# Three 128x9 and 128x4 products move from VectorE to GpSimd, and the splitting of weight parts moves to the end of GpSimd's round

## Chip, core and metric

One core of a Trainium2 chip runs the whole program in one launch. The metric is the device time of that launch in microseconds (us), the median of several runs. The engines are called as in the profile: PE (TensorE; PEld is its weight load), DVE (VectorE), ACT (ScalarE), POOL (GpSimd) and SP (SyncE, which issues the DMAs).

## What is computed

```python
# attention with a memory, B, H, S, D = 4, 8, 576, 64
scores = q @ k^T / sqrt(D), causal
a = exp(scores - max);  a /= a.sum(-1) + 1e-9
local = a @ v
q_p = phi(q)                        # phi(x) = (x if x > 0 else exp(x) - 1) + 1
mem_out = (q_p @ M_prev) / (q_p . z_prev + 1e-6)
g = 1 / (1 + exp(-beta))
x = g * mem_out + (1 - g) * local   # laid out as 2304 tokens x 512
# two dense blocks, d_model 512, d_ff 2048
x = act1(x @ w_in1) @ w_out1        # act1: 0 below -1, h above 1, (h + 1)^2 / 4 between
x = act2(x @ w_in2) @ w_out2        # act2(h) = h * sigmoid(h)
```

## The kernel before

The program has two stages. The first is the attention: 16 rounds, one for each pair of heads p (two heads side by side on the 128 partitions). The second is the two dense blocks, in which PE multiplies in three passes (high and low parts of the operands). No scheduler is at work: each engine's program is written out by hand, and semaphores join them.

**A round of attention.** In round p PE first turns (transposes) the probabilities of pair p: `turn_both` twice and `turn_corner`, nine products at L899 that open the round. Then it forms the scores of pair p+1 (L862), turns more blocks (eleven products at L899, which reuse the PSUM banks of scores), turns phi and the row weights (`turn_rest` with L933 and L934, then `turn_phi` and `turn_row`), and ends with the values and the memory product. The eleven products may start once DVE has taken the maximum of the first scores of pair p+1 out of PSUM (`s_read`).

**DVE's part of iteration p**: the row weights of pair p (`rows`, L674 to L687), `to_x(p-1)` (L711: finished sums times row weight, from PSUM into X), a copy (L704), the masked maxima of pair p+1 (L653), the low parts `klo` (L627) and `qlo` (L635) of pair p+2, and the norms of phi of pair p+1 (`norms`, L659 to L668). All are in that order, so what is late in `rows` delays `to_x` and the maxima behind it.

**The two weights.** With den the row sum of the exponentials (L674), the kernel scales by 1/den only at the end, so phi's weight is den * g / norm. `norms` makes norm (L659), its reciprocal (L664) and times g (L668). `rows` makes den, its reciprocal (L680), den times that share (L685, `rw[:, 1]`), and for the last 64 rows of both heads the small table `rwt` (L687).

**POOL's round p**: `phi_sum_1(p+1)` (L353), `weigh(p)` (L386 and L389: phi times its weight into `phs`), `widen(p)` (L377, L379), in some rounds `split_part` of a weight matrix part (L335, L337), `phi_sum_2` (L358), the high parts `khi` (L344) and `qhi` (L348) of pair p+2, phi times z (L363), and the values times 1 - g (L371). `parts_beside` places one part in each of the rounds 5, 7, 9, 11, 13 and 14 and two in round 15; the other 56 parts are split in the dense stage. A part lands from SP's queue (`fetch`) in one of three slots of `stage`.

Of the kernel before, what the change touches and what calls it, by code (L numbers as in the profile page):

```python
# [7 lines left out]
ALU = mybir.AluOpType  # L8
# [3 lines left out]
P = 128  # L12
# [5 lines left out]
def build(nc, qT, kT, qN, vN, mN, zN, bN, w_in1, w_out1, w_in2, w_out2, out):  # L18
# [6 lines left out]
    PAIRS = NPAIR // B  # L25
    FULL = S // P
# [16 lines left out]
    NB = 2 * FULL + 1  # L43
# [9 lines left out]
    with ExitStack() as ctx:  # L53
        def sem(name):
            return ctx.enter_context(nc.semaphore(name))

        def sb(name, shape, dt=F32, where=ctx):
            return where.enter_context(nc.sbuf_tensor(name, shape, dt))
# [14 lines left out]
        att = ExitStack()  # L73
# [27 lines left out]
        rwide = sb("rwide", [P, 2 * FULL + 2, D], where=att)  # L101
        rwt = sb("rwt", [P, 2, 2], where=att)
        mden = sb("mden", [P, 2, NB], where=att)
        qn = [sb(f"qn{i}", [P, NB, D], where=att) for i in range(2)]
        phie = [sb(f"phie{i}", [P, NB, D + 1], where=att) for i in range(2)]
        phir = [sb(f"phir{i}", [P, NB, D], where=att) for i in range(3)]
# [80 lines left out]
        hi_done, lo_done = sem("hi_done"), sem("lo_done")  # L187
        phi_part, phi_sum, phi_norm = sem("phi_part"), sem("phi_sum"), sem("phi_norm")
        norm_step, row_step, row_wide = sem("norm_step"), sem("row_step"), sem("row_wide")
        weighed, v_done = sem("weighed"), sem("v_done")  # L190
        s_full, s_read, exp_done = sem("s_full"), sem("s_read"), sem("exp_done")
        t_full, ev_act, ev_dve = sem("t_full"), sem("ev_act"), sem("ev_dve")
# [40 lines left out]
        def parts_beside(p):  # L233
            return [u for u, at in enumerate(PARTS_AT) if at == p]
# [92 lines left out]
        def _(pool):  # L327
            def split_part(u):
                layer, f, half = parts[u]
                if layer == 0 and f == EARLY and half == 0:  # L330
                    pool.wait_ge(x_free, NPAIR + 1)
                if layer == 1 and half == 0:
                    pool.wait_ge(g_free, (TILES - 1) * FC + f + 1)
                landed(pool, u)
                nc.gpsimd.tensor_copy(W[f][:, 2 * half, :], stage[:, u % 3, :]).then_inc(w_hi, 1)  # L335
                pool.wait_ge(w_hi, u + 1)
                nc.gpsimd.tensor_tensor(W[f][:, 2 * half + 1, :], stage[:, u % 3, :],  # L337
                                        W[f][:, 2 * half, :].bitcast(F32), ALU.subtract).then_inc(w_split, 1)
# [11 lines left out]
            def phi_sum_1(p):  # L350
                pool.wait_ge(phi_part, 2 * p + 2)
                both = phir[p % 3]
                nc.gpsimd.tensor_tensor(both[:], qn[p % 2][:], both[:], ALU.add).then_inc(phi_sum, 1)  # L353
# [20 lines left out]
            def widen(p):  # L374
                if p:
# [3 lines left out]
                nc.gpsimd.tensor_copy(rwide[:, 0:2 * FULL, :], rw[:, 0, 0:2 * FULL].unsqueeze(2)  # L379
                                      .broadcast_to([P, 2 * FULL, D])).then_inc(row_wide, 1)  # L380

            def weigh(p):
                pool.wait_ge(row_step, 4 * p + 4)
                if p:
                    pool.wait_ge(t_full, TURNS * (p - 1) + T_PHI + 1)
                nc.gpsimd.tensor_tensor(phs[:, 0:2 * FULL, :], phir[p % 3][:, 0:2 * FULL, :],  # L386
                                        rw[:, 1, 0:2 * FULL].unsqueeze(2).broadcast_to([P, 2 * FULL, D]),
                                        ALU.mult).then_inc(weighed, 1)
                nc.gpsimd.tensor_tensor(phs[:, 2 * FULL:, :], phir[p % 3][:, 2 * FULL:, :].broadcast_to([P, 2, D]),  # L389
                                        rwt[:, 1, :].unsqueeze(2).broadcast_to([P, 2, D]),  # L390
                                        ALU.mult).then_inc(weighed, 1)
# [35 lines left out]
            for p in range(NPAIR):  # L427
                if 0 < p < NPAIR - 1:
                    phi_sum_1(p + 1)
                weigh(p)  # L430
                widen(p)

                for u in parts_beside(p):
                    split_part(u)

                if 0 < p < NPAIR - 1:
                    phi_sum_2(p + 1)
                if p + 2 < NPAIR:
                    high_k(p + 2)
                    high_q(p + 2)  # L440
                if p + 1 < NPAIR:
                    phi_times_z(p + 1)
                    weigh_v(p + 1)
            for u in range(2 * EARLY, 4 * FC):
                split_part(u)

# [2 lines left out]
        def _(act):  # L449
# [12 lines left out]
            def phi_part_2(p):  # L462
                act.wait_ge(phi_part, 2 * p + 1)
                if p >= 2:
                    act.wait_ge(norm_step, 3 * p - 5)
                nc.scalar.activation(phie[p % 2][:, :, 0:D], phir[p % 3][:], ACT.Exp, scale=-1.0).then_inc(phi_part, 1)

            def split_x(layer, tile, k_):
# [152 lines left out]
        def _(dve):  # L621
# [34 lines left out]
            def norms(p, step):  # L656
                if step == 0:
                    dve.wait_ge(phi_norm, p + 1)
                    nc.vector.tensor_reduce(mden[:, 0], phie[p % 2][:], AX.X, ALU.add).then_inc(norm_step, 1)  # L659
                elif step == 1:  # L660
                    dve.wait_ge(norm_step, 3 * p + 1)
                    if p:
                        dve.wait_ge(row_step, 4 * p - 1)
                    nc.vector.reciprocal(mden[:, 1], mden[:, 0]).then_inc(norm_step, 1)  # L664
                else:
                    dve.wait_ge(norm_step, 3 * p + 2)
                    dve.wait_ge(gate_step, 5)
                    nc.vector.tensor_tensor(mden[:, 1], mden[:, 1], gcols[:, p % PAIRS, :],  # L668
                                            ALU.mult).then_inc(norm_step, 1)

            def rows(p, step):
                if step == 0:
                    dve.wait_ge(exp_done, NB * p + NB)
                    nc.vector.tensor_scalar(den[:], rowsum[:, p % 2, :], 1e-9, None, ALU.add).then_inc(row_step, 1)  # L674
                    return
                dve.wait_ge(row_step, 4 * p + step)
                if step == 1:
                    if p:
                        dve.wait_ge(t_full, TURNS * p)
                    nc.vector.reciprocal(rw[:, 0, :], den[:]).then_inc(row_step, 1)  # L680
                elif step == 2:
                    dve.wait_ge(norm_step, 3 * p + 3)
                    if p:
                        dve.wait_ge(weighed, 2 * p)
                    nc.vector.tensor_tensor(rw[:, 1, :], den[:], mden[:, 1], ALU.mult).then_inc(row_step, 1)  # L685
                else:
                    nc.vector.tensor_tensor(rwt[:], rw[:, :, 2 * FULL:].broadcast_to([P, 2, 2]),  # L687
                                            bd[:].unsqueeze(1).broadcast_to([P, 2, 2]), ALU.mult).then_inc(row_step, 1)

            def split_x(layer, tile, k_):  # L690
                tok = slice(T0[tile], T0[tile] + TN[tile])
# [43 lines left out]
            for p in range(NPAIR):  # L735
                more, more2 = p + 1 < NPAIR, p + 2 < NPAIR
                if p:
                    for step in range(4):
                        rows(p, step)
                    if more:  # L740
                        to_x(p - 1)
                        empty_second(p)
                    else:
                        empty_second(p)
                        to_x(p - 1)
                if more:
                    for c in range(4):
                        maximum(p + 1, c)
                if p == 0:
                    norms(0, 0)  # L750
                    norms(0, 1)
                    norms(0, 2)
                    for step in range(4):
                        rows(0, step)
                if more:
                    maximum(p + 1, 4)
                empty_main(p, T_M21, 2, 1)
                if more:
                    maximum(p + 1, 5)
                if more:  # L760
                    for c in range(6, 8):
                        maximum(p + 1, c)
                if p == 0:
                    maximum(1, 8)
                    dve.wait_ge(phi_part, 4)
                    nc.vector.tensor_tensor(phir[1][:], qn[1][:], phir[1][:], ALU.add).then_inc(phi_sum, 1)
                    dve.wait_ge(phi_sum, 3)
                    nc.vector.tensor_tensor(phir[1][:], phir[1][:], phie[1][:, :, 0:D], ALU.add).then_inc(phi_sum, 1)
                if more2:
                    low_k(p + 2)  # L770
                if p and more:
                    maximum(p + 1, 8)
                if more2:
                    low_q(p + 2)
                if more:
                    for step in range(3):
                        norms(p + 1, step)
            dve.sem_inc(h_free, H_BANKS)
            for k_ in range(KC):
# [355 lines left out]
```

## Time and profile before

| | |
|---|---|
| time, median of 3 runs | 987.01 us (986.19 to 989.4) |
| the profiled execution | 988.2 us, span 986.1 us |
| busy in the span | PE 975.1, DVE 474.3, ACT 384.1, POOL 285.6 us |
| attention, by PE's round starts | 27.22 us (round 1) to 185.61 us (round 15) |
| dense stage | from 193.62 us (first L1021) to the end |

The busy times alone say that PE is at work nearly all the time. But the ends of matmuls are modelled, so a short wait of PE hides in a longer instruction; round starts tell more. A group named L899 `ps<-ident,prob` is a product with the identity, which turns a block. An operation of DVE or POOL that waits for something other than a semaphore shows as a longer duration, not as idle time: for that its least and its largest duration are to be compared.

### The profile page before, as it was taken

The numbers are of one execution on the slowest core, as the hardware profiler recorded it, in microseconds if no ns is written. First come the engines' busy times: TensorE is split into PE (matmuls) and PEld (weight loads), VectorE is DVE, ScalarE is ACT, GpSimd is POOL, SyncE is SP. The second block draws the span as 40 slices with busy tenths as digits, with TensorE's granted clock in tenths as the row PEclk, the third lists the DMA queues.
The fourth block names the chain that finished last, engine by engine and source line by source line (L and its number), as shares of the span: only waits on it lengthen the run. The fifth ranks groups of instructions, "written<-read, shape, count | busy, mean of one in ns | idle before, by whom it ended". The sixth has DMA issues, their size and how long they took to land.

```text
span 986.1 us, 14130 instructions
## 1 busy us (share of the span) xinstructions
PE 975.1 (99%) x5468; PEld 816.0 (83%) x5468; DVE 474.3 (48%) x946; ACT 384.1 (39%) x847; POOL 285.6 (29%) x304
## 2 busy tenths in 40 slices
PE   7999999999999999999999999999999999999998
PEld 6888877888888888888888998888888888888897
DVE  6999999756344434434434663323332332322232
ACT  6988888633223222322223332322222232222232
POOL 6989999799000000000000798000000000000000
PEclk8999999999999999999999999999999999999999
DMA  6555544244000000000000343001000100100010
GB/s 196 150 157 154 168 145 131 71 119 117 22 1 1 1 0 1 1 1 1 1 1 1 86 129 97 0 1 43 1 1 1 44 0 1 43 1 1 1 44 22
DMA packets 38401, 48.10 MB, mean 49 GB/s; under 512 B 3264, under 2 KB 21696, under 8 KB 38336
## 3 DMA queue, kind: packets, MB, share of 16 engines
q1 hardware_dynamic: 38336, 47.20, 15.9%
q8 instruction: 44, 0.72, 0.3%
q14 instruction: 21, 0.17, 0.1%
HBM read 42.47 MB, written 4.72 MB: 48 GB/s over the span
## 4 chain that ended last, share of the span: by engine, by line
PE 83%; DVE 8%; POOL 3%; issue 2%; ACT 2%; DMA 1%; SPq 0%; POOLq 0%; DVEq 0%
PE ps L1021 26%; PE ps L1023 26%; PE ps L1022 26%; PE ps L899 2%; PE ps L954 1%; DVE prob L653 1%; DVE qlo L635 1%; PE ps L862 1%; DVE ptail L653 1%; DVE mden L659 1%; DVE rw L685 1%; POOL phir L358 1%; ACT prob L476 1%; DVE glo L797 1%; POOL phs L386 1%
## 5 line engine op out<-in xcount | busy, mean ns | idle before, releaser
L1021 PE MATMUL ps<-xhi,W 128*128 128x512 f32 (+1 forms) x640 | 235.4, 368 | 0.0
L1022 PE MATMUL ps<-xlo,W 128*128 128x512 f32 (+1 forms) x640 | 235.4, 368 | 0.0
L1023 PE MATMUL ps<-xhi,W 128*128 128x512 f32 (+1 forms) x640 | 235.4, 368 | 0.0
L797 DVE TENSOR_TENSOR glo<-act_t,ghi 128x512 fp32r<-128x512 f32 (+1 forms) x160 | 118.0, 738 | 223.6 <-ACT ghi L576 223.6
L576 ACT CAST ghi<-act_t 128x512 fp32r<-128x512 f32 (+1 forms) x160 | 92.5, 578 | 235.4 <-PE ps L1023 213.1
L1021 PEld LDWEIGHTS ps<-xhi,W 128*128 128x128 f32 x640 | 120.7, 189 | 20.7
L1022 PEld LDWEIGHTS ps<-xlo,W 128*128 128x128 f32 x640 | 120.6, 188 | 20.4
L1023 PEld LDWEIGHTS ps<-xhi,W 128*128 128x128 f32 x640 | 120.6, 188 | 20.2
L335 POOL CAST W<-stage 128x512 fp32r<-128x512 f32 x64 | 46.2, 722 | 303.0 <-PE ps L1023 300.6
L568 ACT ACTIVATE act_t<-act_t,half_col 128x512 f32<-128x512 f32 (+1 forms) x80 | 54.5, 681 | 185.7 <-DVE act_t L790 185.7
L1021 PE MATMUL ps<-ghi,W 128*128 128x512 f32 (+1 forms) x320 | 118.1, 369 | 0.3 <-DVE glo L797 0.2
L1022 PE MATMUL ps<-glo,W 128*128 128x512 f32 (+1 forms) x320 | 117.7, 368 | 0.0
L1023 PE MATMUL ps<-ghi,W 128*128 128x512 f32 (+1 forms) x320 | 117.7, 368 | 0.0
L1021 PE MATMUL ps<-W,glo 128*128 128x512 f32 x288 | 112.2, 390 | 0.0
L1022 PE MATMUL ps<-W,ghi 128*128 128x512 f32 x288 | 112.2, 390 | 0.0
L1023 PE MATMUL ps<-W,ghi 128*128 128x512 f32 x288 | 112.0, 389 | 0.0
L795 DVE TENSOR_TENSOR act_t<-ps,act_t 128x512 f32<-128x512 f32 (+1 forms) x80 | 51.0, 637 | 110.2 <-ACT act_t L572 110.1
L572 ACT ACTIVATE act_t<-ps 128x512 f32<-128x512 f32 (+1 forms) x80 | 44.4, 555 | 118.6 <-PE ps L1023 118.4
L337 POOL TENSOR_TENSOR W<-stage,W 128x512 fp32r<-128x512 f32 x64 | 86.1, 1345 | 5.1
L792 DVE TENSOR_TENSOR act_t<-ps,act_t 128x512 f32<-128x512 f32 (+1 forms) x80 | 51.1, 638 | 59.8 <-ACT act_t L568 59.8
L790 DVE TENSOR_SCALAR act_t<-ps 128x512 f32<-128x512 f32 (+1 forms) x80 | 50.7, 634 | 57.4 <-PE ps L1023 57.4
L476 ACT ACTIVATE prob<-prob,negmax 128x128 f32<-128x128 f32 (+3 forms) x128 | 71.3, 568 | 5.4 <-DVE negmax L653 5.4
(113 smaller groups left out, 1336.5 us busy)
## 6 DMA issues: line engine op xcount, KB each, us to landing
stage<-in_moe_w_in SPq DMA_DIRECT2D x32, 256.0 KB, 2.7
stage<-in_moe_w_out SPq DMA_DIRECT2D x32, 256.0 KB, 2.7
vn<-in_vN SPq DMA_DIRECT2D x16, 320.0 KB, 5.0
qraw<-in_qT SPq DMA_DIRECT2D x15, 320.0 KB, 3.2
qn<-in_qN SPq DMA_DIRECT2D x16, 288.0 KB, 4.9
zb<-in_zN SPq DMA_DIRECT2D x32, 144.0 KB, 3.6
out_x<-ostage SPq DMA_DIRECT2D x17, 256.0 KB, 2.0
kraw<-in_kT SPq DMA_DIRECT2D x15, 288.0 KB, 2.9
```

The costliest lines, as they stand in the source:

```text
L335: nc.gpsimd.tensor_copy(W[f][:, 2 * half, :], stage[:, u % 3, :]).then_inc(w_hi, 1)
L337: nc.gpsimd.tensor_tensor(W[f][:, 2 * half + 1, :], stage[:, u % 3, :], W[f][:, 2 * half, :].bitcast(F32), ALU.subtract).then_inc(w_split, 1)
L476: nc.scalar.activation(a, a, ACT.Exp, bias=negmax[:, p % 2, c:c + 1], scale=-1.0, accum_out=rowsum[:, p % 2, c:c + 1]).then_inc(exp_done, 1)
L568: nc.scalar.activation(a, a, ACT.Square, bias=half_col[:], scale=0.5).then_inc(a_act, 1)
L576: nc.scalar.copy(ghi[:, f % SLOTS, 0:TN[tile]], a).then_inc(ghi_done, 1)
L790: nc.vector.tensor_scalar(a, h, -1.0, 1.0, ALU.max, ALU.min).then_inc(a_dve, 1)
L792: nc.vector.tensor_tensor(a, h, a, ALU.max).then_inc(h_free, 1)
L795: nc.vector.tensor_tensor(a, h, a, ALU.mult).then_inc(h_free, 1)
L797: nc.vector.tensor_tensor(glo[:, f % SLOTS, 0:TN[tile]], a, ghi[:, f % SLOTS, 0:TN[tile]].bitcast(F32), ALU.subtract).then_inc(glo_done, 1)
L1021: nc.tensor.matmul(dst, w_lo_, x_hi_, start=first, stop=False)
L1022: nc.tensor.matmul(dst, w_hi_, x_lo_, start=False, stop=False)
L1023: return nc.tensor.matmul(dst, w_hi_, x_hi_, start=False, stop=last)
```

## The change

`norms` loses its last step and `rows` its last two. POOL does them as `shares(p)` (mden times gcols, 128x9), and `weights(p)` (den times share, 128x9, and the table rwt, 128x4), between `phi_sum_1(p+1)` and `weigh(p)`. A new tile `share` and two semaphores, `gated` and `row_made`, join them. The splitting of parts moves from behind `widen` to the end of POOL's round, behind the values of L371. In round 0 DVE forms the row weights before the norms.

```diff
+            def shares(p):
+                pool.wait_ge(norm_step, 2 * p + 2)
+                if p == 0:
+                    pool.wait_ge(gate_step, 5)
+                nc.gpsimd.tensor_tensor(share[:], mden[:, 1], gcols[:, p % PAIRS, :], ALU.mult).then_inc(gated, 1)
+
+            def weights(p):
+                pool.wait_ge(gated, p + 1)
+                pool.wait_ge(row_step, 2 * p + 1)
+                nc.gpsimd.tensor_tensor(rw[:, 1, :], den[:], share[:], ALU.mult).then_inc(row_made, 1)
+                pool.wait_ge(row_step, 2 * p + 2)
+                pool.wait_ge(row_made, 2 * p + 1)
+                nc.gpsimd.tensor_tensor(rwt[:], rw[:, :, 2 * FULL:].broadcast_to([P, 2, 2]),
+                                        bd[:].unsqueeze(1).broadcast_to([P, 2, 2]), ALU.mult).then_inc(row_made, 1)
+
             def weigh(p):
-                pool.wait_ge(row_step, 4 * p + 4)
+                pool.wait_ge(row_made, 2 * p + 2)
...
+                shares(p)
+                weights(p)
                 weigh(p)
                 widen(p)
-
-                for u in parts_beside(p):
-                    split_part(u)
...
                     weigh_v(p + 1)
+                for u in parts_beside(p):
+                    split_part(u)
...
                 if step == 0:
                     dve.wait_ge(phi_norm, p + 1)
                     nc.vector.tensor_reduce(mden[:, 0], phie[p % 2][:], AX.X, ALU.add).then_inc(norm_step, 1)
-                elif step == 1:
-                    dve.wait_ge(norm_step, 3 * p + 1)
+                else:
+                    dve.wait_ge(norm_step, 2 * p + 1)
                     if p:
-                        dve.wait_ge(row_step, 4 * p - 1)
+                        dve.wait_ge(gated, p)
                     nc.vector.reciprocal(mden[:, 1], mden[:, 0]).then_inc(norm_step, 1)
-                else:
-                    dve.wait_ge(norm_step, 3 * p + 2)
-                    dve.wait_ge(gate_step, 5)
-                    nc.vector.tensor_tensor(mden[:, 1], mden[:, 1], gcols[:, p % PAIRS, :],
-                                            ALU.mult).then_inc(norm_step, 1)
...
                 if step == 0:
                     dve.wait_ge(exp_done, NB * p + NB)
+                    if p:
+                        dve.wait_ge(row_made, 2 * p)
...
-                elif step == 2:
-                    dve.wait_ge(norm_step, 3 * p + 3)
-                    if p:
-                        dve.wait_ge(weighed, 2 * p)
-                    nc.vector.tensor_tensor(rw[:, 1, :], den[:], mden[:, 1], ALU.mult).then_inc(row_step, 1)
-                else:
-                    nc.vector.tensor_tensor(rwt[:], rw[:, :, 2 * FULL:].broadcast_to([P, 2, 2]),
-                                            bd[:].unsqueeze(1).broadcast_to([P, 2, 2]), ALU.mult).then_inc(row_step, 1)
```

How POOL's instructions stand from the widening of round 5 to the weighing of round 6, before (bracketed are the semaphores that each waits for):

```order
L379 COPY rwide<-rw 128x512
L335 CAST W<-stage 128x512 [waits w_in0_0]
L337 TENSOR_TENSOR W<-stage,W 128x512 [waits w_hi]
L358 TENSOR_TENSOR phir<-phir,phie 128x576 [waits phi_sum]
L344 CAST khi<-kraw 128x576 [waits s_full,k_in1]
L348 CAST qhi<-qraw 128x640 [waits q_in1]
L363 TENSOR_TENSOR phie<-phir,zb 128x9x64 [waits z_in,phi_sum]
L371 TENSOR_TENSOR vn<-vn,local 128x640 [waits v_in0]
L353 TENSOR_TENSOR phir<-qn,phir 128x576 [waits phi_part]
L386 TENSOR_TENSOR phs<-phir,rw 128x512 [waits t_full,row_step]
```

The same stretch in the changed program, whose line numbers are 2 or more higher:

```order
L381 COPY rwide<-rw 128x512
L360 TENSOR_TENSOR phir<-phir,phie 128x576 [waits phi_sum]
L346 CAST khi<-kraw 128x576 [waits s_full,k_in1]
L350 CAST qhi<-qraw 128x640 [waits q_in1]
L365 TENSOR_TENSOR phie<-phir,zb 128x9x64 [waits z_in,phi_sum]
L373 TENSOR_TENSOR vn<-vn,local 128x640 [waits v_in0]
L337 CAST W<-stage 128x512 [waits w_in0_0]
L339 TENSOR_TENSOR W<-stage,W 128x512 [waits w_hi]
L355 TENSOR_TENSOR phir<-qn,phir 128x576 [waits phi_part]
L388 TENSOR_TENSOR share<-mden,gcols 128x9 [waits norm_step]
L393 TENSOR_TENSOR rw<-den,share 128x9 [waits row_step,gated]
L396 TENSOR_TENSOR rwt<-rw,bd 128x4 [waits row_made,row_step]
L403 TENSOR_TENSOR phs<-phir,rw 128x512 [waits t_full,row_made]
```

The split has moved behind the values, and three small products stand between the sum of phi and its weighing, each waiting for the one ahead of it.

DVE's instructions from the last low part of iteration 3 to the copy behind `to_x`, before:

```order
L635 TENSOR_TENSOR qlo<-qraw,qhi 128x640 [waits hi_done]
L659 TENSOR_REDUCE mden<-phie 128x9 [waits phi_norm]
L664 RECIPROCAL mden<-mden 128x9 [waits row_step,norm_step]
L668 TENSOR_TENSOR mden<-mden,gcols 128x9 [waits gate_step,norm_step]
L674 TENSOR_SCALAR den<-rowsum 128x9 [waits exp_done]
L680 RECIPROCAL rw<-den 128x9 [waits t_full,row_step]
L685 TENSOR_TENSOR rw<-den,mden 128x9 [waits weighed,norm_step,row_step]
L687 TENSOR_TENSOR rwt<-rw,bd 128x4 [waits row_step]
L711 TENSOR_TENSOR X<-ps,turned 128x576 [waits ev_act,values_done]
L704 COPY probT<-ps 128x2x2x128 [waits t_full]
```

And in the changed program:

```order
L653 TENSOR_TENSOR qlo<-qraw,qhi 128x640 [waits hi_done]
L677 TENSOR_REDUCE mden<-phie 128x9 [waits phi_norm]
L682 RECIPROCAL mden<-mden 128x9 [waits gated,norm_step]
L689 TENSOR_SCALAR den<-rowsum 128x9 [waits row_made,exp_done]
L694 RECIPROCAL rw<-den 128x9 [waits t_full,row_step]
L717 TENSOR_TENSOR X<-ps,turned 128x576 [waits ev_act,values_done]
L710 COPY probT<-ps 128x2x2x128 [waits t_full]
```

The three products are gone from DVE, and `to_x` stands right behind the reciprocal of the row sums.

## Rows read from the trace of the kernel before

A row of the trace in order of time begins with the start and the duration in us.

**Rows 1.** Busy time by stretch, then PE clock, DMA share, GB/s
```profile
100.00:120.00 20.00, 19.61 (x194) 15.95 (x195) 18.93 (x52) 17.90 (x52) 18.85 (x20) 1.00 0.44 135
...
260.00:400.00 140.00, 140.00 (x619) 115.97 (x618) 59.14 (x87) 39.29 (x60) 0.00 (x0) 1.00 0.00 1
```

**Rows 2.** TensorE in order of time: rounds 1, 4, 5 and 15
```profile
27.22 1.20 PE L899 MATMUL ps<-ident,prob 128*128 128x128 f32 x9
...
60.88 1.20 PE L899 MATMUL ps<-ident,prob 128*128 128x128 f32 x9
...
64.24 1.42 PE L899 MATMUL ps<-ident,prob 128*128 128x128 f32 x11
...
71.94 1.20 PE L899 MATMUL ps<-ident,prob 128*128 128x128 f32 x9
...
185.61 1.20 PE L899 MATMUL ps<-ident,prob 128*128 128x128 f32 x9
...
188.40 0.36 PE L933 MATMUL ps<-sident,phs 128*128 128x64 f32 x2
```

**Rows 3.** TensorE in order of time: rounds 10 and 11
```profile
128.41 1.20 PE L899 MATMUL ps<-ident,prob 128*128 128x128 f32 x9
...
132.38 1.42 PE L899 MATMUL ps<-ident,prob 128*128 128x128 f32 x11 [0.40 <-DVE negmax L653]
...
140.08 1.20 PE L899 MATMUL ps<-ident,prob 128*128 128x128 f32 x9
```

**Rows 4.** VectorE in order of time: round 9 into 10
```profile
128.53 0.18 DVE L668 TENSOR_TENSOR mden<-mden,gcols 128x9 f32<-128x9 f32 x1
128.63 0.16 DVE L674 TENSOR_SCALAR den<-rowsum 128x9 f32<-128x9 f32 x1
...
129.08 1.01 DVE L685 TENSOR_TENSOR rw<-den,mden 128x9 f32<-128x9 f32 x1
...
130.21 0.75 DVE L711 TENSOR_TENSOR X<-ps,turned 128x576 f32<-128x576 f32 x1
```

**Rows 5.** GpSimd in order of time: rounds 8 and 9
```profile
107.65 1.05 POOL L386 TENSOR_TENSOR phs<-phir,rw 128x512 f32<-128x512 f32 x1 [0.30 <-DVE rwt L687]
...
115.47 2.00 POOL L353 TENSOR_TENSOR phir<-qn,phir 128x576 f32<-128x576 f32 x1
118.32 1.05 POOL L386 TENSOR_TENSOR phs<-phir,rw 128x512 f32<-128x512 f32 x1 [0.85 <-DVE rwt L687]
119.33 0.40 POOL L389 TENSOR_TENSOR phs<-phir,rwt 128x128 f32<-128x128 f32 x1
119.67 0.29 POOL L377 COPY rwide<-rwt 128x128 f32<-128x128 f32 x1
...
120.47 0.61 POOL L335 CAST W<-stage 128x512 fp32r<-128x512 f32 x1
121.16 1.28 POOL L337 TENSOR_TENSOR W<-stage,W 128x512 fp32r<-128x512 f32 x1
...
128.65 1.41 POOL L353 TENSOR_TENSOR phir<-qn,phir 128x576 f32<-128x576 f32 x1
130.37 1.05 POOL L386 TENSOR_TENSOR phs<-phir,rw 128x512 f32<-128x512 f32 x1 [0.31 <-DVE rwt L687]
```

**Rows 6.** GpSimd in order of time: rounds 0, 14 and 15
```profile
28.62 1.43 POOL L353 TENSOR_TENSOR phir<-qn,phir 128x576 f32<-128x576 f32 x1 [1.27 <-ACT phie L466]
...
175.90 1.05 POOL L386 TENSOR_TENSOR phs<-phir,rw 128x512 f32<-128x512 f32 x1 [0.30 <-DVE rwt L687]
...
182.76 1.27 POOL L371 TENSOR_TENSOR vn<-vn,local 128x640 f32<-128x640 f32 x1
186.57 1.05 POOL L386 TENSOR_TENSOR phs<-phir,rw 128x512 f32<-128x512 f32 x1 [2.54 <-DVE rwt L687]
```

**Rows 7.** Single lines: least, median and largest duration, first and last start
```profile
L416 POOL MEMSET bd<- x2: 92/92/93, 4.7 to 4.9; 64x1 f32 x2
...
L685 DVE TENSOR_TENSOR rw<-den,mden x16: 168/171/1017, 17.8 to 186.1; 128x9 f32<-128x9 f32 x16
```

More of the change, by code:

```diff
@@ L103, in build @@
         mden = sb("mden", [P, 2, NB], where=att)
+        share = sb("share", [P, NB], where=att)
         qn = [sb(f"qn{i}", [P, NB, D], where=att) for i in range(2)]
@@ L189, in build @@
         norm_step, row_step, row_wide = sem("norm_step"), sem("row_step"), sem("row_wide")
+        gated, row_made = sem("gated"), sem("row_made")
         weighed, v_done = sem("weighed"), sem("v_done")
@@ L464, in phi_part_2 @@
                 if p >= 2:
-                    act.wait_ge(norm_step, 3 * p - 5)
+                    act.wait_ge(norm_step, 2 * p - 3)
                 nc.scalar.activation(phie[p % 2][:, :, 0:D], phir[p % 3][:], ACT.Exp, scale=-1.0).then_inc(phi_part, 1)
@@ L673, in rows @@
                     dve.wait_ge(exp_done, NB * p + NB)
+                    if p:
+                        dve.wait_ge(row_made, 2 * p)
                     nc.vector.tensor_scalar(den[:], rowsum[:, p % 2, :], 1e-9, None, ALU.add).then_inc(row_step, 1)
-                    return
-                dve.wait_ge(row_step, 4 * p + step)
-                if step == 1:
+                else:
+                    dve.wait_ge(row_step, 2 * p + 1)
                     if p:
@@ L737, in _ @@
                 if p:
-                    for step in range(4):
+                    for step in range(2):
                         rows(p, step)
@@ L749, in _ @@
                 if p == 0:
+                    for step in range(2):
+                        rows(0, step)
                     norms(0, 0)
                     norms(0, 1)
-                    norms(0, 2)
-                    for step in range(4):
-                        rows(0, step)
                 if more:
@@ L775, in _ @@
                 if more:
-                    for step in range(3):
+                    for step in range(2):
                         norms(p + 1, step)
```

## The prediction

> **What bounds the kernel now.** I first read busy time by stretch [rows 1]. Past 260 us PE is busy for all of 140 us: the dense stage is PE's, and no edit touches it. In the attention stage PE, DVE and POOL are all busy for some 19 of 20 us, so the page can't say which one sets the pace. For that I read PE's round starts in order of time. From round 4 to round 5 PE takes 71.94 - 60.88 = 11.06 us [rows 2] without a pause; I call 11.05 PE's own round. Round 10 takes 140.08 - 128.41 = 11.67 us [rows 3], and PE is seen waiting there for a maximum of DVE before its eleven products of L899. Over rounds 1 to 14 PE needs 185.61 - 27.22 = 158.39 us [rows 2], and 14 x 11.05 is 154.70. So **3.69 us** are lost. They are the only thing in this stage that an edit to DVE can give back.
>
> Why is DVE late? In order of time [rows 4] L685, 9 columns wide, takes 1.01 us, though its median is 171 ns and its least 168 [rows 7]. It starts at 129.08 and ends at 130.09. POOL's L353 runs from 128.65 to 130.06 [rows 5]. So this product of two SBUF operands stands until POOL's instruction is over. It then pushes `to_x` (L711) to 130.21 and the maxima behind it. PE's eleven products start at 132.38, 2.17 us after L711; in an undisturbed round they start at 64.24 - 60.88 = 3.36 us into the round. So L711 may start up to 3.36 - 2.17 = 1.19 us into PE's round. In round 10 it starts at 130.21 - 128.41 = 1.80, and 0.61 us are lost, which is the 11.67 less 11.05 with 0.01 over. L685 has this long form in rounds 2, 6, 8, 10, 12 and 14, the six rounds that lose: 3.69 / 6 is 0.61.
>
> And POOL? From L386 of round 8 to the end of L353 it works from 107.65 to 117.47, 9.82 us; in round 9, with a split part, from 118.32 to 130.06, 11.74 us [rows 5]. Then it waits 0.85 and 0.31 us for DVE's `rwt`. Two such rounds are 21.56 us of work against PE's 22.10.
>
> **The change, part by part.**
>
> *DVE.* Three products go from each of 16 rounds. Without L668, den (L674) can start at 128.53 instead of 128.63; L711 followed L674 by the start of the product at 129.08 - 128.63 = 0.45, so it would start at 128.98, not 130.21. That is 0.57 us into PE's round, under the 1.19. In round 2 and in the rounds behind a split, DVE as such stops delaying PE. The ceiling of the gain is 3.69 us. The moved split points the same way: L344 comes 1.92 us (11.74 - 9.82) earlier after L386, and in a round with a split L711 now comes 128.98 - 118.32 - 1.92 = 8.74 us after it.
>
> *POOL.* Each of the three products costs its time plus the handover to the next, since each waits for the one before. No row shows a 128x9 product on POOL, so I bound it. L386 with 512 columns takes 1.05 us and L389 with 128 takes 0.40, which is 1.69 ns a column; 9 columns give 0.40 - 119 x 0.00169 = 0.20 us. The handover is that of L337 behind L335: 121.16 - (120.47 + 0.61) = 0.08 us [rows 5]. I call the sum c and take 0.28 us, since L386 and L389 are products with a broadcast operand as the new ones are. The low end is the fill L416 with one column, 0.09 us [rows 7], and the same handover, c = 0.17; nothing at all is excluded, because each must end before the next begins. The high end is L389 itself, unshortened, c = 0.48. All three lie on POOL's own path. The first needs no handover from L353, which it overlaps by about 0.05 us (L389 overlaps L386 by 0.04, L377 overlaps L389 by 0.06).
>
> POOL's round is thus 9.78 + 3c without a split and 11.70 + 3c with one, at 0.28 10.62 and 12.54. **Two rounds are 23.16 us, against PE's 22.10.** POOL has become the slower engine wherever every second round has a part.
>
> *The lag that POOL may run up.* POOL's results aren't needed at once. `phs` and the first widening must be ready when PE comes to L933. In round 15 that is 188.40 - 185.61 = 2.79 us into PE's round [rows 2], and only there so early, since no scores stand ahead of it. From the start of L386 to the end of L377 are 119.67 + 0.29 - 118.32 = 1.64 us [rows 5], and I estimate 0.04 for the signal to PE: 1.68 (now it is 188.40 - 186.57 = 1.83, which bounds it). So I follow POOL from round 1 to round 15 without idle time. In round 1 its L353 ends at 28.62 + 1.43 [rows 6], where it had waited for ACT: 30.00 after the overlap. From there:
>
> - round 1's three products: 30.00 + 3c
> - eight rounds without a split (1 to 4, 6, 8, 10, 12): 8 x (9.78 + 3c)
> - five with one (5, 7, 9, 11, 13): 5 x (11.70 + 3c)
> - round 14, which has no high parts but a split: from 175.90 to the end of L371, 182.76 + 1.27 [rows 6], less 0.05: 8.08 + 3c
>
> L386 of round 15 starts at 174.82 + 45c, with c = 0.28 at 187.42, and L933 at 189.10. It starts at 188.40 now. The loss that DVE caused is gone, and POOL's is 0.70 larger. That POOL has no idle time in rounds 2 to 5 holds as long as L386 stays behind den: with c = 0.28 it starts 73.32 - 71.94 = 1.4 us into round 5, and den is there earlier.
>
> *The rest.* The two added waits of DVE (`gated` at L682, `row_made` at L689) are for products that POOL did a round before: nothing. Behind them stands `to_x`, and PE waits for that; if POOL were a whole round late they would cost. The split at the round's end holds up SP's `fetch` of later parts, behind which no load of attention stands in the last rounds; parts 6 and 7 of round 15 are needed well after the first L1021: nothing. In round 0 DVE's exchanged order makes `phs` some 0.2 us later, PE's L933 waits for others there: nothing.
>
> **Sum.** Gain 3.69, loss 3.69 + 0.70: the profiled execution of 988.2 us would become 988.9. It stands 1.2 us above the median of the runs, which is 987.01, so the median becomes 987.7 us. In general the difference is 174.82 + 45c + 1.68 - 188.40 = 45c - 11.90, never under -3.69. Each 0.01 us in c is 0.45 us.
>
> The Trainium skill, "GPSIMD Engine Reference", section "Performance versus the Vector engine", speaks against the move: a two-input elementwise product takes GpSimd 1.96 times as long as VectorE, measured at 2048 columns. No row here shows a product of 9 columns on GpSimd. By that ratio on L685's 0.171 us a product would take 0.335 us, and the sum would be +6.8 us.
>
> **Rivals.**
>
> 1. *POOL's small products cost no more than a fill.* At c under 0.20 the sum passes -2.96 us, 0.3% of the time. The six delays go and no lag takes their place: at the ceiling 983.3 us. For it speaks the fill's 0.09 us; against it that both products in the trace put the part that doesn't grow with columns at 0.18 or so. 0.10.
> 2. *Slower: the price is high.* Small products may not lie on the line through L386 and L389. With c = 0.42, halfway and more from 0.28 to L389's own 0.48, POOL's two rounds take 24.00 us and the lag grows by 1.90 a pair: 45 x 0.42 - 11.90 = +7.0, 994.0 us. It decides from c = 0.33 on (+2.95). For it speaks that the last two products wait for two semaphores each, against it that L386 waits for two as well. The ratio of the skill's page above ends beside it. 0.17.
> 3. *The change doesn't free DVE.* L711 too could stand until L353 is over. It would then start at about 130.1, as now; the six losses stay beside POOL's work. POOL's chain is then still what ends last, and the time is that of the forecast or up to 1 us above, 988.7. 0.05, within 0.3%.
> 4. *Forecast:* POOL sets the end, c from 0.20 to 0.33, 984 to 990 us. 0.68.
>
> Faster, same and slower by 0.3% (2.96 us, about what a measurement of this kernel can tell from no change) are 0.10, 0.73 and 0.17. The range of 8 in 10 goes from c = 0.19, 983.8, to c = 0.355, 991.1; its low end can't be much lower, because of the ceiling.
>
> **What would show it.** Right: POOL's idle time before L386 (now L403) is gone, the three products start 0.28 us apart, and L403 starts at about 73.3 in round 5 and 187.4 in round 15. DVE has no 1.01 us product of 9 columns. PE's rounds 2 and 6 take 11.05, while rounds 9, 11 and 13 lose about 1 us each to a maximum that waited for `khi`, and L933 of round 15 waits for POOL some 0.9 us. Wrong: another pitch of the small products (the most likely miss), or idle time of POOL that I have left out.

## The result, and the profile after

| | before | changed |
|---|---|---|
| median of 14 runs | 986.86 us (985.96 to 989.4) | 988.69 us (987.81 to 991.21) |
| ratio, 95% interval | | 1.0022 (1.0015 to 1.0029) |

The kernel became slower by 0.22%, which is 2.2 us (1.5 to 2.9) by the ratio. That is within 0.3%, in the direction that was forecast, and three times the 0.7 us of the forecast.

The page first, the busy times of the changed kernel and its chain of waits by engine:

```profile
PE 974.7 (99%) x5468; PEld 815.8 (83%) x5468; DVE 464.1 (47%) x898; ACT 385.1 (39%) x847; POOL 295.5 (30%) x352
...
PE 84%; POOL 9%; ACT 2%; DVE 2%; issue 2%; DMA 0%; SPq 0%; POOLq 0%
```

DVE's busy time is 10.2 us less than before, POOL's 9.9 us more, and POOL now has 9% of the chain where it had 3%. Next PE in order of time, the changed kernel's rounds 9 and 10 and its last, and the first product of the dense stage:

```profile
115.34 1.20 PE L904 MATMUL ps<-ident,prob 128*128 128x128 f32 x9
...
119.04 1.42 PE L904 MATMUL ps<-ident,prob 128*128 128x128 f32 x11 [0.28 <-DVE negmax L671]
...
126.74 1.20 PE L904 MATMUL ps<-ident,prob 128*128 128x128 f32 x9
...
133.39 0.41 PE L938 MATMUL ps<-sident,phs 128*128 128x64 f32 x2 [0.65 <-DVE negmax L671]
...
138.66 1.20 PE L904 MATMUL ps<-ident,prob 128*128 128x128 f32 x9
...
185.30 1.20 PE L904 MATMUL ps<-ident,prob 128*128 128x128 f32 x9
...
188.99 0.41 PE L938 MATMUL ps<-sident,phs 128*128 128x64 f32 x2 [0.74 <-POOL rwide L379]
...
194.26 0.50 PE L1026 MATMUL ps<-xhi,W 128*128 128x512 f32 x1
```

These rows answer to [rows 2, 3]; in the changed kernel L904 is L899 of before, L938 is L933, L671 is L653, L403 is L386, L355 is L353 and L717 is L711. Round 9 takes 126.74 - 115.34 = 11.40 us and round 10 11.92 us, 23.32 together, where two of PE's own rounds are 22.10 and rounds 10 and 11 of the kernel before took 22.72 (11.67 and 11.05). PE now waits at two places. One is the old one, a maximum of DVE ahead of the eleven products: they start 119.04 - 115.34 = 3.70 us into round 9, 0.34 later than in a round of PE's own (3.36). The other is new, L938, which needs `phs`. In the last round the trace names POOL there. In round 10 it names DVE, whose maxima had been done 0.65 us before; PE goes on after POOL's first widening is ready, 1.64 us after L403's start at 131.61 (below). Next POOL, L403 of round 1, then rounds 8 to 10, then L403 of round 15:

```profile
29.54 1.05 POOL L403 TENSOR_TENSOR phs<-phir,rw 128x512 f32<-128x512 f32 x1
...
108.29 1.05 POOL L403 TENSOR_TENSOR phs<-phir,rw 128x512 f32<-128x512 f32 x1
...
116.69 1.43 POOL L355 TENSOR_TENSOR phir<-qn,phir 128x576 f32<-128x576 f32 x1
118.09 0.20 POOL L388 TENSOR_TENSOR share<-mden,gcols 128x9 f32<-128x9 f32 x1
118.36 0.21 POOL L393 TENSOR_TENSOR rw<-den,share 128x9 f32<-128x9 f32 x1
118.71 0.20 POOL L396 TENSOR_TENSOR rwt<-rw,bd 128x4 f32<-128x4 f32 x1
118.99 1.05 POOL L403 TENSOR_TENSOR phs<-phir,rw 128x512 f32<-128x512 f32 x1
...
131.61 1.05 POOL L403 TENSOR_TENSOR phs<-phir,rw 128x512 f32<-128x512 f32 x1
...
187.21 1.04 POOL L403 TENSOR_TENSOR phs<-phir,rw 128x512 f32<-128x512 f32 x1
```

There is no idle time in brackets on any row, against 0.30 and 0.85 us in [rows 5]. POOL's two rounds are 131.61 - 108.29 = 23.32 us, the same as PE's: PE goes at POOL's pace. DVE, too, waits longer for POOL's high part `khi` (0.50 us at most before, from round 1 on), and so it is late with what follows, `to_x` and the maximum of round 9 among it:

```profile
112.41 1.24 DVE L645 TENSOR_TENSOR klo<-kraw,khi 128x576 fp32r<-128x576 f32 x1 [2.01 <-POOL khi L346]
```

The three products take 0.20, 0.21 and 0.20 us, and start to start 0.27, 0.35 and 0.28; over all rounds the first of these is 0.27 to 0.31 and the others hardly move.

The two profiled executions can't be compared by their spans (986.1 and 986.7 us). The granted clock of PE in the start-up differs. The columns are stretch, its length, busy time of PE, PEld, DVE, ACT and POOL, then clock, DMA share and GB/s. First the changed kernel:

```profile
10.00:15.00 5.00, 4.08 (x30) 3.36 (x30) 3.60 (x16) 5.00 (x19) 4.84 (x5) 0.74 0.86 267
15.00:20.00 5.00, 4.35 (x35) 3.65 (x31) 4.93 (x20) 4.24 (x14) 3.47 (x8) 0.91 0.64 207
```

And the kernel before, run once more (experiment e1):

```profile
10.00:15.00 5.00, 4.13 (x27) 3.36 (x28) 3.30 (x12) 5.00 (x19) 4.84 (x5) 0.66 0.88 271
15.00:20.00 5.00, 5.00 (x32) 4.25 (x31) 4.21 (x21) 3.04 (x8) 3.21 (x5) 0.66 0.73 205
```

The clock is a mean over its two levels, 1.2 and 2.4 GHz, and between 15 and 20 us the lower one holds longer in e1. Round 1 of PE starts at 25.84 us in the one and at 27.22 [rows 2] in the other. So times are compared by the ratio of many runs, and traces by what lies after the start of round 1. From there to the first product of the dense stage the changed kernel takes 194.26 - 25.84 = 168.42 us and the one before 193.62 - 27.22 = 166.40 [rows 2]: 2.02 us more. From that product to the last one both take 788.8 us.

### The profile page after: what moved, and what is told of

Its sections match the earlier page's. It is cut to its first block, busy times and chain, and to the rows that moved or that the text cites. A ratio compares the mean times of both kernels' runs of the same rounds, so it can differ in the third digit from the quotient of the medians.

```text
span 986.7 us, 14146 instructions
## 1 busy us (share of the span) xinstructions
PE 974.7 (99%) x5468; PEld 815.8 (83%) x5468; DVE 464.1 (47%) x898; ACT 385.1 (39%) x847; POOL 295.5 (30%) x352
## 4 chain that ended last, share of the span: by engine, by line
PE 84%; POOL 9%; ACT 2%; DVE 2%; issue 2%; DMA 0%; SPq 0%; POOLq 0%
PE ps L1026 26%; PE ps L1027 26%; PE ps L1028 26%; PE ps L959 2%; POOL phie L365 2%; POOL vn L373 2%; PE ps L867 1%; PE ps L904 1%; POOL phs L403 1%; POOL phir L360 1%; ACT prob L494 1%; DVE glo L802 1%; POOL phir L355 1%; PE ps L979 1%; POOL W L339 1%
## 5 line engine op out<-in xcount | busy, mean ns | idle before, releaser
L337 POOL CAST W<-stage 128x512 fp32r<-128x512 f32 x64 | 46.0, 719 | 303.0 <-PE ps L1028 300.5
```

## The experiments

Ratios are to the kernel before, run in turn on the same chip, with 95% intervals. Differences between two experiments are formed from their ratios.

**e1, the kernel before once more.** No edit.

> The kernel before, unchanged, to read its trace in an execution whose granted clock doesn't fall in the first 20 us. Ratio 1.000. The six PE rounds of 11.6 to 11.8 us should be there again with L685 at 1.01 us; round 1 should start some 1.3 us earlier than the 27.22 us of the profile shown, as the changed kernel's did (25.84), and the last L933 about 1.9 us earlier than the changed kernel's (188.99), at about 187.1. If round 1 starts at 27.2 here too, the start-up gain belongs to the change and not to the clock.

Ratio 1.0002 (0.9992 to 1.0011). The six long rounds are there again (11.6 to 11.8 us, L685 at 1.01 or 1.02). Its trace again had the low clock at the start, and round 1 started at 27.02 us, so by itself it can't tell the clock from the change. Two later traces can. With a clock of 0.83 over 10 to 20 us e2, and with 1.00 e7, start round 1 at 25.90 and 24.87 us though neither has the change in the products; e3, which has it, starts at 27.63 with 0.66. The early start goes with the clock and not with the change. The first product of its dense stage:

```profile
193.50 0.49 PE L1021 MATMUL ps<-xhi,W 128*128 128x512 f32 x1
```

That is the reference for any trace with this start.

**e2, only the split moves.** In POOL's round:

```diff
                 widen(p)
-                for u in parts_beside(p):
-                    split_part(u)
...
                     weigh_v(p + 1)
+                for u in parts_beside(p):
+                    split_part(u)
```

> Only the split moves to the end of GpSimd's round; the three products stay on VectorE. Theory (GpSimd's chain with three products sets the end; the split's place doesn't matter to its sum): L685 still meets L353 behind every split and stands about 1 us, so the same six rounds lose 0.6 us each: ratio 0.9995 to 1.0005. Rival (khi 1.9 us earlier in a split round is what frees VectorE): up to 3.7 us faster, 0.9965.

Ratio 1.0005 (0.9996 to 1.0013). The product den times share on DVE (least, median and largest ns), and the start of the dense stage:

```profile
L684 DVE TENSOR_TENSOR rw<-den,mden x16: 169/171/1018, 17.6 to 186.0; 128x9 f32<-128x9 f32 x16
```

```profile
193.45 0.49 PE L1020 MATMUL ps<-xhi,W 128*128 128x512 f32 x1
```

The long form is still there, in five of the six rounds (6, 8, 10, 12 and 14; round 2 has the short one in this execution, whose round 1 took 12.61 us), and the dense stage starts within 0.05 us of e1's. The split's place is worth nothing that can be measured, as the theory said; the rival is out.

**e3, only the products move.** The split goes back behind `widen`, all else as changed:

```diff
                 widen(p)
+                for u in parts_beside(p):
+                    split_part(u)
...
                     weigh_v(p + 1)
-                for u in parts_beside(p):
-                    split_part(u)
```

> Only the three products move to GpSimd; the split stays behind widen. Theory: GpSimd has the same work without idle time, L403 of round 15 starts within 0.5 us of the changed kernel's 187.2, ratio to before 1.002 as for the whole change. Rival (the split's new place holds up GpSimd's next phs and is what costs): back to 1.000 or under. Second rival (with the split early, khi is late by 1.9 us and VectorE's to_x is past its limit): 1 to 3 us slower than the changed kernel, 1.004.

Ratio 1.0026 (1.0016 to 1.0036): the whole change's cost within both intervals. The products alone make it. The clock of its start was as low as e1's (0.70 and 0.62 between 10 and 20 us):

```profile
188.89 1.05 POOL L403 TENSOR_TENSOR phs<-phir,rw 128x512 f32<-128x512 f32 x1
...
195.94 0.50 PE L1027 MATMUL ps<-xhi,W 128*128 128x512 f32 x1
```

The dense stage starts 195.94 - 193.50 = 2.44 us after e1's; 0.61 us of it lie ahead of round 1 (27.63 against 27.02). L403 is at 188.89 and not within 0.5 us of 187.2, as was expected: the start-up was later. From round 1 (31.33) it takes 157.56 us, and the changed kernel 157.67, so POOL's pace is the same. The second rival was half right: with the split early PE does wait for `to_x` (0.27 us idle, four times), but within POOL's pace, and the time isn't the 1.004 it gave.

**e4, one product less on POOL.** The first product goes back to DVE, with semaphores to match:

```diff
-                nc.gpsimd.tensor_tensor(share[:], mden[:, 1], gcols[:, p % PAIRS, :], ALU.mult).then_inc(gated, 1)
...
+                    nc.vector.tensor_tensor(mden[:, 1], mden[:, 1], gcols[:, p % PAIRS, :],
+                                            ALU.mult).then_inc(norm_step, 1)
```

> The changed kernel with the first product (mden times gcols) back on VectorE; the other two and the split as changed. Theory: GpSimd's chain is 15 x 0.29 = 4.4 us shorter, so L403 of round 15 is no longer what ends last but PE nearly so: 2.0 to 2.6 us faster than before, ratio 0.9975, and 4 us faster than the changed kernel. Rival (VectorE's stalls on the shared access, now at den, are what costs): it keeps them and stays at 1.001 to 1.002.

Ratio 0.9983 (0.9974 to 0.9992): 1.7 us faster than before and 3.8 faster than the changed kernel.

```profile
185.46 0.41 PE L936 MATMUL ps<-sident,phs 128*128 128x64 f32 x2 [0.61 <-POOL rwide L378]
...
190.74 0.50 PE L1024 MATMUL ps<-xhi,W 128*128 128x512 f32 x1
```

POOL still sets the end of attention (0.61 us idle ahead of the last L936), but the dense stage starts 194.26 - 190.74 = 3.52 us earlier than in the changed kernel. The rival, that DVE's stalls are what costs, is out: this version keeps them, den takes 0.84, 1.33 and 1.27 us in rounds 4, 7 and 15. It is 0.3 us short of the least gain expected, and the trace shows where more than that went: POOL now waits for den four times, 0.17 to 0.25 us each, the first in round 4:

```profile
59.86 0.20 POOL L386 TENSOR_TENSOR rw<-den,mden 128x9 f32<-128x9 f32 x1 [0.17 <-DVE den L686]
```

Its L396, the weighing, takes 154.61 us from round 1 to round 15 where the terms without the first product give 144.82 + 14 x 0.63 = 153.64.

**e5, one product more on POOL.** Behind the first product, which now writes `share0`, in the same chain:

```diff
+                pool.wait_ge(gated, 2 * p + 1)
+                nc.gpsimd.tensor_tensor(share[:], share0[:], ones[:], ALU.mult).then_inc(gated, 1)
```

> The changed kernel with a fourth 128x9 product on GpSimd each round (share times ones), in the same chain ahead of phs. Theory (GpSimd has no idle time from round 1 to 15 and sets the end): 15 x 0.28 = 4.2 us more, L403 of round 15 at 191.4 plus up to 1.4 by the clock of the first 20 us; ratio to before 1.0065. Rival (VectorE's stalls or PE set the end and GpSimd only hangs behind): 0 to 1 us more, 1.002 to 1.003.

Ratio 1.0071 (1.0057 to 1.0085), 4.8 us over the changed kernel. POOL's chain in round 10:

```profile
133.43 0.20 POOL L390 TENSOR_TENSOR share<-mden,gcols 128x9 f32<-128x9 f32 x1
133.71 0.21 POOL L392 TENSOR_TENSOR share<-share,ones 128x9 f32<-128x9 f32 x1
134.00 0.21 POOL L397 TENSOR_TENSOR rw<-den,share 128x9 f32<-128x9 f32 x1
134.35 0.20 POOL L400 TENSOR_TENSOR rwt<-rw,bd 128x4 f32<-128x4 f32 x1
134.63 1.05 POOL L407 TENSOR_TENSOR phs<-phir,rw 128x512 f32<-128x512 f32 x1
```

The added product takes 0.29 us from its start to the next, and 15 x 0.29 is 4.4. From round 1 to round 15 L407 takes 4.13 us more than L403 did, 14 x 0.295. POOL sets the end, at full price for each operation of 9 columns.

**e6, e7 and e8, other rounds for the parts.** One line, in the changed kernel (e6), in the kernel before (e7) and in e4 (e8):

```diff
-        PARTS_AT = [5, 7, 9, 11, 13, 14, 15, 15]
+        PARTS_AT = [7, 11, 13, 14, 15, 15, 15, 15]
```

> The changed kernel with parts split in rounds 7, 11, 13, 14 and four in round 15 instead of 5, 7, 9, 11, 13, 14 and two. Theory: 2 x 1.92 us of GpSimd's work leave the chain that sets the end: 3.0 to 3.9 us faster than the changed kernel, ratio to before 0.9985. Rival (the parts 4 to 7 come too late for the dense stage): PE waits for a part after 194 us, ratio 1.002 or more.

> The kernel before with the same new places of the parts. Theory: the rounds behind a split are four instead of six with the one at round 2, each 0.61 us: 1.2 us faster, ratio 0.9988. Rival (the 1.01 us form of the product isn't tied to the splits): 1.000.

> Two products on GpSimd, the first on VectorE, the split last, and the new places of the parts. Theory: GpSimd's two rounds are under PE's 22.10 us nearly everywhere, so PE's own round sets the pace: 1.5 to 2.3 us faster than with the old places, ratio to before 0.9960 to 0.9975. Rival (VectorE's sum of the row sums now meets L353 and stands): PE rounds of 11.3 to 11.5 us, 0.998.

e6: ratio 0.9994 (0.9985 to 1.0003), 2.8 us under the changed kernel, a little under the 3.0 to 3.9 expected. Two splits of 1.92 us left the chain, and most of it came back as time.

e7: 0.9993 (0.9984 to 1.0002), 0.7 us where 1.2 were expected; the interval holds both and no change too. Its trace says more:

```profile
24.87 1.20 PE L899 MATMUL ps<-ident,prob 128*128 128x128 f32 x9
...
182.08 1.20 PE L899 MATMUL ps<-ident,prob 128*128 128x128 f32 x9
...
190.09 0.49 PE L1021 MATMUL ps<-xhi,W 128*128 128x512 f32 x1
...
192.72 0.50 PE L1021 MATMUL ps<-xhi,W 128*128 128x512 f32 x1 [0.28 <-DVE xlo L693]
```

L685 is long in four rounds (2, 8, 12 and 14), and rounds 1 to 14 take 157.21 us where they took 158.39: the 1.2 us are there. But the dense stage got longer. From its first product to its last are 789.4 us in the traces of e6, e7, e8 and e9, against 788.8 in all the others. No part of a weight came too late. PE waits for DVE's low parts of X (L693), and four of those take 5.11 us in e7 where they take 3.60 in e1; POOL's extra splits now run beside them. So the new places of the parts cost 0.6 us, which none of the expectations had.

e8: 0.9976 (0.9968 to 0.9985). That is 0.7 us faster than e4, where 1.5 to 2.3 were expected, and it is nearer to the rival's 0.998. From round 1 to the dense stage 163.92 us are left of e4's 165.08, and 0.6 of the gain is lost in the dense stage. The rival's sign is there too: den stands in rounds 3, 9, 10 and 13 (0.86 to 1.39 us). In the two where it ends latest, 1.3 us into round 3 and 1.4 into round 13, the rounds take 11.33 and 11.44 us. Rounds 1 and 14 take 11.31 and 11.25 without it. Its den on DVE:

```profile
L686 DVE TENSOR_SCALAR den<-rowsum x16: 158/167/1387, 15.3 to 180.9; 128x9 f32<-128x9 f32 x16
```

**e9, den without the form that stands.** In e8, the sum with a constant becomes a reduction over pairs of a row sum and 1e-9 (`rowsum` gets a last dimension of 2, whose second half is set once):

```diff
-                    nc.vector.tensor_scalar(den[:], rowsum[:, p % 2, :], 1e-9, None, ALU.add).then_inc(row_step, 1)
+                    nc.vector.tensor_reduce(den[:], rowsum[:, p % 2], AX.X, ALU.add).then_inc(row_step, 1)
```

> The kernel of e8 with den formed by a sum over pairs (row sum, 1e-9) in place of the sum with a constant, since of VectorE's small operations the reduction of L659 never stood behind GpSimd and the one with a constant now does (up to 1.39 us). Theory: den takes under 0.3 us in every round, the PE rounds of 11.3 us at its places become 11.05, 0.5 to 1.1 us faster than e8, ratio to before 0.9968. Rival (some other operation meets L353 instead): 0.9976 as e8.

Ratio 0.9970 (0.9959 to 0.9980), median 983.07 us. It is the fastest kernel of this study, 3.0 us under the one before. Its den, and two of its PE rounds:

```profile
L687 DVE TENSOR_REDUCE den<-rowsum x16: 158/171/174, 15.9 to 180.6; 128x9 f32<-128x18 f32 x16
```

```profile
147.38 1.20 PE L903 MATMUL ps<-ident,prob 128*128 128x128 f32 x9
...
158.43 1.20 PE L903 MATMUL ps<-ident,prob 128*128 128x128 f32 x9
```

158.43 - 147.38 is 11.05, and all rounds of its attention are like this one. By time alone e8 and e9 can't be told apart (their intervals overlap); by the trace the stalls of den are gone, and rounds 3 and 13 take 11.05. Four of the new reductions start while POOL's L354 is running, and each takes 0.17 us. From round 1 to the dense stage this kernel takes 188.58 - 25.84 = 162.74 us, 3.66 less than the kernel before: the whole of the 3.69 us that the prediction called lost, of which the dense stage takes 0.6 back. The 3.0 us by the ratio agree.

**e10, the order of two waits.** In the changed kernel:

```diff
+                pool.wait_ge(row_made, 2 * p + 1)
                 pool.wait_ge(row_step, 2 * p + 2)
-                pool.wait_ge(row_made, 2 * p + 1)
```

> The changed kernel with the two waits ahead of rwt's product in the other order, the one on GpSimd's own product first. The third product starts 0.35 us after the second where the second starts 0.29 after the first. If the order of the waits makes that difference, the 0.35 becomes 0.28 and 15 x 0.07 = 1.0 us are gained on the changed kernel, ratio to before 1.0011; if the form of the operand does, nothing changes, 1.0022.

Ratio 1.0012 (1.0003 to 1.0021), 1.0 us under the changed kernel. POOL in round 10:

```profile
130.51 0.20 POOL L388 TENSOR_TENSOR share<-mden,gcols 128x9 f32<-128x9 f32 x1
130.79 0.21 POOL L393 TENSOR_TENSOR rw<-den,share 128x9 f32<-128x9 f32 x1
131.07 0.20 POOL L396 TENSOR_TENSOR rwt<-rw,bd 128x4 f32<-128x4 f32 x1
131.35 1.05 POOL L403 TENSOR_TENSOR phs<-phir,rw 128x512 f32<-128x512 f32 x1
```

All three products now start 0.28 us apart, in every round, and L403 takes 156.75 us from round 1 to round 15 where it took 157.67: 0.92 less, 14 x 0.07. The program's order of two waits is worth 0.07 us a round: the wait that is met last is the one to put first. The times alone don't show it, since the two intervals overlap.

## Why the prediction was right, and where its size was off

- **PE's own round, the 3.69 us lost, and their cause** held. e2 keeps L685's long form and the time; e9 has neither it nor den's, runs at 11.05 us throughout, and its trace gives back 3.66 us before the dense stage.
- **POOL becomes the slower engine** held: no idle time from L355 of round 1 to round 15, two rounds of 23.32 us where 23.16 were forecast. From round 1 to the dense stage the traces show 4.4 us more with one product more on POOL (e5), 3.3 less with one less (e4), and 3.7 less with two splits less (e6).
- **The formula 45c - 11.90** held in form. From L403 of round 1 to that of round 15 the trace has 187.21 - 29.54 = 157.67 us; the sum of the prediction's terms is 144.82 + 14 x 3c, 157.70 with the measured 3c = 0.92. (At the low end of the range, c = 0.19, the formula gives 983.7 and not 983.8.)
- **The mis-sized term is c.** Its parts, 0.20 us a product and 0.08 us of handover, were right for two of the three. The third started 0.35 us after the second. So the three cost 0.92 us and not 3 x 0.28 = 0.84, c is 0.307, and 15 x 0.08 = 1.2 us bring the sum from +0.7 to +1.9. e10 takes the cause away and is left with 1.2 us over the kernel before (0.3 to 2.1), where the prediction with its c of 0.28 had 0.7. The handover was read from L337 behind L335, which has a single wait; what a second wait costs, and that their order counts, no row of before showed.
- **The signal to PE** took 188.99 - 187.21 = 1.78 us from L403 to L938, where 1.68 was estimated: 0.1 us.
- **"DVE has no 1.01 us product of 9 columns"** was right, but *DVE is freed* wasn't quite. den took the place of L685. DVE in order of time, rounds 4 to 5 and 8 to 9 of the changed kernel:

```profile
70.14 1.35 DVE L689 TENSOR_SCALAR den<-rowsum 128x9 f32<-128x9 f32 x1 [0.25 <-ACT ptail L494]
...
71.66 0.71 DVE L717 TENSOR_TENSOR X<-ps,turned 128x576 f32<-128x576 f32 x1
...
116.45 0.30 DVE L689 TENSOR_SCALAR den<-rowsum 128x9 f32<-128x9 f32 x1
...
116.92 0.71 DVE L717 TENSOR_TENSOR X<-ps,turned 128x576 f32<-128x576 f32 x1
```

and POOL beside the first of them:

```profile
70.05 1.42 POOL L355 TENSOR_TENSOR phir<-qn,phir 128x576 f32<-128x576 f32 x1
```

den stands from 70.14 to 71.49, until POOL's L355 is over at 71.47, and L717 follows at 71.66, 1.57 us into PE's round (70.09). With 1.19 allowed, PE's eleven products come 0.33 us late there (73.78 - 70.09 = 3.69, against 3.36). In round 6 den takes 1.20 us, and the round 11.24. In the changed kernel this hides behind POOL's lag, so it adds nothing to the sum. In e8, where POOL doesn't set the pace, the same form of den goes with PE rounds of 11.33 and 11.44 us, and e9 has neither. The prediction's third rival had such a stall, but put it at `to_x`.
- **Where PE loses the time** came out otherwise in part. Rounds 9, 11 and 13 were to lose 1 us each to a maximum that waited for `khi`. They lose 0.35 that way, and rounds 10, 12 and 14 lose 0.87 at L938, which the prediction expected to be early enough in every round but the last. In round 15 PE waits there 0.74 us where 0.9 were forecast. The sum doesn't depend on this, since it follows POOL.
- **The rival of a high price** (c from 0.33) was the nearest of the rivals, but the measured c of 0.307 lies in the forecast's own 0.20 to 0.33. The ratio of 1.96 of the Trainium skill, "GPSIMD Engine Reference", section "Performance versus the Vector engine", which the page measured for an add of 2048 columns, wasn't reached: 0.207 us on GpSimd against 0.171 on VectorE is 1.2, at 9 columns.
- **L403 at 187.4 in round 15**: it was 187.21, but that is luck: two errors met there, 1.2 us of c and the 1.4 us by which round 1 started earlier in this execution. For the same reason L403 of round 5 was at 72.34 and not at 73.3.

What stays open: some 0.2 us between +2.0 by the terms, which is also what the two traces show, and 2.2 by the ratio; the interval doesn't tell it from nothing. Why two waits cost more when the late one stands last isn't shown either, only that they do.

## What to carry to other kernels

- When three engines are each some 95% busy, sum what a *round* costs on each and compare with the bottleneck's own round. An engine with 0.3 us of idle time in one round and 0.8 in the next can't take 0.9 us more in each, however small the operations are.
- Small operations that wait for each other cost their time plus the handover, in full, on a saturated engine; moving two of three was faster by 0.17%, moving all three slower by 0.22%.
- A stall is removed by the form of the instruction that stands (e9), not only by moving it to another engine.
- Work that is moved out of one stage is to be priced in the next: two parts moved from rounds 5 and 9 to round 15 took 1.2 us off the attention of e7 and put 0.6 us on its dense stage.

## What the runs showed of the hardware

- On VectorE a product of two SBUF operands and the sum with a constant, both of 9 columns, stand until a running GpSimd instruction ends (1.02 and 1.39 us where 0.17 is usual); the reciprocal and the reduction didn't (0.21 to 0.22 us and 0.75 to 0.77 us beside POOL's instructions in every trace, and den as a reduction 0.174 us at most in 16). The Trainium skill, "SBUF — State Buffer", section "Who interferes with whom", says that `tensor_scalar` may enter a mode with both ports, that two SBUF inputs contend with a GpSimd that reads, and that `tensor_reduce` never contends on trn2. These traces agree.
- On GpSimd the order of two waits ahead of an instruction changed its start by 0.07 us (0.35 against 0.28 after the one before).
- The granted clock between 10 and 20 us, in stretches of 5 us, was 0.62 to 0.98 in some traces and 1.00 in others (e6, e7, e8); from 20 us on it is 1.00 in all of them. Of e1's runs those with a clock of 1.000 over the whole span took 985.5 to 985.9 us and those with 0.997 988.1 to 988.5: the start-up moves the time by as much as the change does. The changed kernel's runs with 1.000 took 987.8 to 988.7 us, so at a like clock none of them overlaps with e1's.
